# Two tiles of one expert's rows between attention and the expert loop, in place of one: picked from eight token tiles, their second matrix in plain float32

## The reference, cut to what matters

```python
scores = scale * q @ k.T, masked to 0 <= i - j < 64          # batch 4, heads 8, seq 576, head_dim 64
x = softmax(scores) @ v                                      # as x[2304, 512]
logits = x @ w_gate + log1p(exp(x @ w_noise)) * noise        # [2304, 8]
top2, top2_w = the two largest of each row, softmax over the two
for e in range(8):
    for k in range(2):
        mask = top2[:, k] == e
        h = np.maximum(x[mask] @ w1[e], 0.0)                 # w1[e]: 512 x 1024
        out[mask] += top2_w[mask, k, None] * (h @ w2[e])     # w2[e]: 1024 x 512
g = ramp(out @ w_in)                                         # 512 x 2048, piecewise quadratic
result = g @ w_out                                           # 2048 x 512
```

## Time and profile before

| | |
|---|---|
| time, median of 3 runs | 1076.76 us (1076.67 to 1077.49) |
| the profiled execution's own time | 1075.81 us |
| its span in the profile | 1073.8 us |
| mean granted TensorE clock | 0.998 |
| PE busy | 1054.0 us, 98% of the span |
| DVE, ACT, POOL busy | 344.5, 357.4, 392.9 us |

### The profile page before, as it was taken

How to read it: one execution, slowest core, us unless ns; L and a number is a source line. 1 busy time by engine, 2 the same in 40 slices (tenths; PEclk the granted TensorE clock), 3 DMA queues, 4 the chain that set the end, 5 groups by cost and what they waited for, 6 DMA issues and landing times.

```text
span 1073.8 us, 17646 instructions
## 1 busy us (share of the span) xinstructions
PE 1054.0 (98%) x5848; PEld 880.8 (82%) x5849; DVE 344.5 (32%) x695; ACT 357.4 (33%) x829; POOL 392.9 (37%) x309
## 2 busy tenths in 40 slices
PE   8999979999999999999999999999999999999998
PEld 6988758888888888888888887988888888888886
DVE  5878841122211221112221122332333332333222
ACT  4668532222222222222222221533344334335333
POOL 6233188785917255280552807830010000100000
PEclk9999999999999999999999999999999999999999
DMA  7685655949633324132241412240021002101001
GB/s 198 185 261 177 208 160 178 349 157 356 211 117 117 117 98 156 39 123 112 90 164 39 162 54 69 93 123 20 20 56 43 20 3 77 40 1 40 1 1 40
DMA packets 49282, 120.08 MB, mean 112 GB/s; under 512 B 6160, under 2 KB 11408, under 8 KB 48720
## 3 DMA queue, kind: packets, MB, share of 16 engines
q0 software_dynamic: 16688, 62.66, 17.7%
q1 hardware_dynamic: 19008, 32.62, 9.8%
q10 hardware_dynamic: 13536, 24.12, 6.6%
HBM read 86.88 MB, written 32.51 MB: 111 GB/s over the span
## 4 chain that ended last, share of the span: by engine, by line
PE 92%; DVE 2%; ACT 2%; DMA 1%; issue 1%; another core or an unknown queue 1%; ACTq 0%; POOL 0%; SPq 0%; DVEq 0%; POOLq 0%
PE bank L1521 7%; PE bank L1519 7%; PE bank L1520 7%; PE bank L1502 7%; PE bank L1504 7%; PE bank L1503 7%; PE bank L1567 6%; PE bank L1569 6%; PE bank L1568 6%; PE bank L1560 6%; PE bank L1562 6%; PE bank L1561 6%; PE bank L1527 3%; PE bank L1290 2%; PE bank L1486 2%; PE bank L1316 2%
## 5 line engine op out<-in xcount | busy, mean ns | idle before, releaser
L487 POOL TENSOR_TENSOR Wl<-stage,Wh 128x2048 fp32r<-128x2048 f32 x36 | 165.8, 4606 | 3.0
L1167 DVE COPY y_out<-bank 128x512 f32<-128x512 f32 x42 | 29.1, 692 | 353.8 <-PE bank L1521 353.8
L1502 PE MATMUL bank<-Wh,xT_h 128*128 x336 | 135.3, 403 | 1.3 <-issue 0.8
L1205 DVE SCALAR_TENSOR_TENSOR bank<-bank,square 128x512 f32<-128x512 f32 x72 | 50.4, 700 | 254.9 <-ACT square L839 254.9
L1504 PE MATMUL bank<-Wh,xT_l 128*128 x336 | 131.4, 391 | 0.0
L1521 PE MATMUL bank<-Wh,hT_l 128*128 x336 | 131.1, 390 | 0.0
L1519 PE MATMUL bank<-Wh,hT_h 128*128 x336 | 130.8, 389 | 0.1
L1520 PE MATMUL bank<-Wl,hT_h 128*128 x336 | 130.7, 389 | 0.0
L1503 PE MATMUL bank<-Wl,xT_h 128*128 x336 | 130.7, 389 | 0.0
L810 ACT ACTIVATE hT_h<-bank 128x512 fp32r<-128x512 f32 x84 | 45.7, 596 | 246.7 <-PE bank L1527 230.2
L485 POOL CAST Wh<-stage 128x2048 fp32r<-128x2048 f32 x36 | 68.5, 1904 | 157.9 <-PE bank L1521 156.5
(11 more groups left out here) (237 smaller groups left out, 1733.7 us busy)
## 6 DMA issues: line engine op xcount, KB each, us to landing
stage<-w POOLq DMA_DIRECT2D x32, 1024.0 KB
y_sorted<-y_out ACTq DMA_DIRECT2D x42, 256.0 KB
x_in<-x_sorted ACTq DMA_DIRECT2D x38, 256.0 KB
x_sorted<-gath_b SPq DMA_DIRECT2D x20, 256.0 KB
v_ring<-vW SPq DMA_DIRECT2D x36, 128.0 KB, 4.5
x_rows<-x_blk SPq DMA_DIRECT2D x36, 128.0 KB, 3.0
x_sorted<-gath_a SPq DMA_DIRECT2D x18, 256.0 KB
k_ring<-kT SPq DMA_DIRECT2D x8, 512.0 KB, 5.4
```

The costliest lines, as they stand in the source:

```text
L487: nc.gpsimd.tensor_tensor(Wl[:, s, cols], stage[:, c % 2], Wh[:, s, cols], ALU.subtract).then_inc(w_ready, 1)
L1502: nc.tensor.matmul(H_ps[a][:], xT_h[:, u, k], high, start=(k == 0), stop=False)
```

## The change

`EARLY` becomes 8 token tiles and the early tiles become two (`FIRST` = 2), of up to 256 rows of the star. `TILES` falls from 42 to 41, `ALL_TILES` stays 43.

- The steps of the early routing move from attention steps 13 to 26 to steps 20 to 35, with tiles twice as wide, four more matmuls in `early_ranks` and in `early_tokens` and a few more small operations. `BY_SCALAR` falls from 11 steps to 8, all of them even.
- The weights of the star are loaded from POOL's step 29 on (before: 23), w2 into a landing buffer of its own, `late_raw`. Only the 8 pieces of w1 are cast and split before routing; those of w2 are split after `find_tokens`, for the tiles of the loop.
- `early_out` multiplies with w2 as it landed: 8 matmuls in float32 for each of the two tiles, where it was 24 in fp32r for one. The hidden rows are copied once, without a low part.
- PE's order between attention and loop changes; all three fillers there are gone.
- The second expert's splitting waits for both early tiles to be stored and for all pieces of the star.

```diff
-BY_SCALAR = (15, 16, 17, 19, 20, 21, 22, 23, 26, 29, 32)
+BY_SCALAR = (20, 22, 24, 26, 28, 30, 32, 34)
+CASTS = {30: (0, 1), 31: (1, 2), 32: (2, 4), 33: (4, 5), 34: (5, 7), 35: (7, 8)}
+LOWS = {32: (0, 2), 34: (2, 4), 36: (4, 5), 37: (5, 6), 38: (6, 8)}
...
-    TILES = ALL_TILES - 1
+    FIRST = 2
+    TILES = ALL_TILES - FIRST
-    EARLY = E // 2
+    EARLY = E * FIRST // 2
...
+            late_raw = sb("late_raw", [P, 2 * STG])
+            e_hT = sb("e_hT", [P, FIRST, KF, P])
...
                 if t == GB:
-                    pool.wait_ge(ey_stored, 16)
+                    pool.wait_ge(ey_stored, 16 * FIRST)
+                    pool.wait_ge(w_ready, 4)
                     first_parts(1, 1, 1)
...
+            def early_hidden(b, first, after):
                 for i in range(first, after):
...
+                    if b == 0 and i in (0, KD):
+                        pe.wait_ge(w_ready, 1 + i // KD)
...
+            def early_out(b, first, after):
+                for k in range(first, after):
+                    if b == 0 and k % 4 == 0:
+                        pe.wait_ge(late_staged[k // 4], 16)
                     if k % 4 == 0:
-                        pe.wait_ge(ehl_ready, 1 + k // 4)
-                    cols = slice(KD * FF + D * k, KD * FF + D * k + D)
-                    for r, (h, w) in enumerate(((e_hT_h, Wh), (e_hT_h, Wl), (e_hT_l, Wh))):
-                        mm = nc.tensor.matmul(EY_ps[:], h[:, k], w[:, 0, cols], start=(k == 0 and r == 0),
-                                              stop=(k == KF - 1 and r == 2))
-                mm.then_inc(ey_done, 1)
+                        pe.wait_ge(ehT_copied, 2 * b + 1 + k // 4)
+                    mm = nc.tensor.matmul(EY_ps[b][:], e_hT[:, b, k], late_raw[:, D * k:D * k + D], start=(k == 0),
+                                          stop=(k == KF - 1))
...
                 if s == G + 1:
-                    pe.wait_ge(w_ready, 2)
-                    pe.wait_ge(exh_ready, 1)
-                    early_hidden(0, 2)
+                    early_transposes(1)
                 if s == G + 3:
-                    early_hidden(2, 4)
+                    early_hidden(0, 0, 4)
                 if s == G + 4:
-                    early_hidden(4, 8)
+                    early_hidden(0, 4, 8)
...
-            keep_busy(banks[0], 5)
+            early_hidden(0, 8, 24)
+            early_turn(0, 0)
+            early_hidden(1, 0, 12)
+            early_turn(0, 1)
             pe.wait_ge(route, ROUTE_PICKED)
...
-            early_out()
+            early_hidden(1, 12, 24)
+            pe.wait_ge(x_ready, G)
+            early_out(0, 0, 6)
...
-            keep_busy(banks[0], 8)
-            pe.wait_ge(tables_ready, 1)
-            pe.wait_ge(ey_copied, 1)
+            for a in range(2):
+                early_turn(1, a)
+            early_out(0, 7, 8)
...
+            early_out(1, 0, 4)
             transpose_x(0, 0, 0)
-            keep_busy(banks[0], 6)
+            early_out(1, 4, 8)
+            pe.wait_ge(tables_ready, 1)
+            pe.wait_ge(ey_copied, 1)
             tile_step(0, 0, 0)
```

More of the change, by code:

```diff
@@ L752, in _ @@
                 step(s)
-            for k in range(G + 4 - 24, 4 * PIECES):
-                cast_piece(k)
             act.wait_ge(route, ROUTE_NEGABS)
@@ L779, in _ @@
                 nc.scalar.activation(oh_lo[:, c], col_sq[:, k % 2], ACT.Relu, scale=-1.0, bias=1.0).then_inc(act_onehots, 1)
-            act.wait_ge(ey_done, 1)
-            nc.scalar.activation(e_y[:], EY_ps[:], ACT.Copy).then_inc(ey_copied, 1)
-            act.wait_ge(ey_copied, 1)
-            act.dma_start(y_sorted[0:P], e_y[:]).then_inc(ey_stored, 16)
+            for a in range(2):
+                early_turned(1, a)
+            for k in range(2 * PIECES, 3 * PIECES):
+                cast_piece(k)
+            early_y(0)
             act.wait_ge(ids_done, 1)
@@ L815, in tile_step @@
                     fetch(t + 4, u)
-            for u in range(2):
-                high_x(u, u)
+            high_x(0, 0)
+            for k in range(3 * PIECES, 4 * PIECES):
+                cast_piece(k)
+            early_y(1)
+            high_x(1, 1)
             act.wait_ge(y_cleared, 16 * (ALL_TILES - SURE))
@@ L1046, in step @@
                 early_step(s)
-                if 25 <= s < G:
-                    low_piece(s - 25)
+                for k in range(*LOWS.get(s, (0, 0))):
+                    low_piece(k)
             for s in range(G + 3):
@@ L1066, in _ @@
             nc.vector.memset(picked[:, NT], 0.0).then_inc(zeroed, 1)
-            for k in range(G - 25, 4 * PIECES):
-                low_piece(k)
+            early_then(nc.vector.tensor_tensor(order_eq[:], order_f[0:1].unsqueeze(2).to_broadcast([1, E, E]),
+                                               place[0:1, 0].unsqueeze(1).to_broadcast([1, E, E]), ALU.is_equal))
             dve.wait_ge(const_ready, ALL_CONSTANTS)
@@ L1146, in _ @@
             then(nc.vector.tensor_reduce(end_by_place[:], end_at[:], AX_X, ALU.add))
-            then(nc.vector.tensor_copy(last_tile[:], end_by_place[:]))
+            then(nc.vector.tensor_scalar(last_tile[:], end_by_place[:], 1.0 - FIRST, None, ALU.add))
             dve.wait_ge(route_act, 3)
```

240 lines of the change are left out of this document (131 added, 109 removed).

## The result

| | kernel before | changed kernel |
|---|---|---|
| time, median | 1077.12 us (1074.83 to 1078.03, 6 runs) | 1087.34 us (1083.98 to 1088.74, 6 runs) |
| the profiled execution | span 1073.8 | 1088.41, span 1086.8 |

The ratio is 1.0082 (95% interval 1.0065 to 1.01): 8.8 us slower by this ratio and 10.2 by the medians, where 8.7 us faster was forecast. The steps that the sum names for attention and for the stretch behind it can be found in the trace, most of them near their price. What is not in the sum is in the loop and the dense layer, whose instructions the change leaves as they were.

What follows compares the result with a forecast made beforehand. PE, busy 98%, was taken to bound the kernel, with DVE's routing chain and the gather bounding the stretch before the loop. -12.25 - 1.1 + 1.8 + 2.85 = -8.7 gave 1068.1 us, range 1065.2 to 1070.8.

Steps and rivals of the forecast that it cites:

- D: Rival: second expert's weights, started late by POOL, hold up the loop; 1083 at a slip to 190; chance 0.02.
- Part 1: Loop: one tile fewer, all tiles costing the same on PE; -12.25 us.
- Part 2: Attention: even steps no longer stalled, -1.5; more PE matmuls, +0.2; DVE's level steps, +0.2; in all -1.1 us.
- Part 3: Last scores to last logits: DVE's added pieces delay hidden matmuls, with the logits queued behind; +1.8 us, bounds 0.9 and 2.3.
- Part 4: Last logits to loop: float32 matmuls at 0.87 us fill PE's idle time; +2.85 us, bounds 0.4 and 3.5.
- rival A: Float32 matmuls ahead of the loop take two passes, 0.456 us each; that stretch +0.4, time 1065.6; chance 0.10.
- Part 5: Gathers in attention and the second expert's splitting cost nothing; gathers issued near 99.5 and 103.7, with 2.5 us margin.
- Rival E: PE's clock sinks under float32 work; 5 us at half rate would cost 2.5, 1070.6; chance 0.05.
- the forecast's case: The main sum holds: 1066.6 to 1069.8 us; chance 0.60.

Runs made afterwards that it cites:

- a1: The changed kernel with an unused 32-byte tensor behind `e_token`, restoring the loop's and dense layer's old SBUF addresses: 1064.39 us, again 1065.41 us.
- c4: a1 with the last logits put ahead of the four hidden matmuls `early_hidden(0, 4, 8)`: 1065.27 us, again 1064.87 us.
- b1: The kernel before without its unused 32-byte tensor `spare`, nothing else changed: 1097.11 us, ratio 1.0182.
- a3: The changed kernel with a 32-byte gap right ahead of `xT_h`, so only the loop's operands are back at multiples of 128 bytes: 1073.36 us.
- d1: a1 without `early_out(1, 0, 4)`, the first four of the second early tile's eight float32 matmuls: 1067.47 us.
- c1: The changed kernel with gaps ahead of `Wh` and the early tiles' tensors: `Wh`, `Wl` 32 bytes off, `xT`, `hT`, `gT`, `zT` at old places: 1084.39 us.
- e0: The changed kernel itself, run once more beside a1 on one chip: 1085.34 us.

## Why the prediction was wrong

**The step that failed** is the first one: "All tiles cost the same on PE", taken over from before to after, and with it the silent zero for the dense layer. Neither holds, since the change moved one operand of each of these matmuls by 32 bytes against the other. A tile takes 12.51 us in place of 12.25, which is 10.7 us over 41 tiles, and the dense layer 9 us more. None of the rivals was this. D, the only one that came out slower, had the second expert's weights; they did not hold anything up. In the changed kernel's trace POOL starts them at 156.51 (forecast 152), and PE's gaps in the loop are 0.25, 0.69 and 0.61 us, none of them put down to POOL or these weights.

**What was right** shows in a1, which is the change without the shifted addresses. The forecast was 1068.1 (1065.2 to 1070.8); a1 took 1064.39, which is 0.8 below the range, and 1065.41, which is in it. So even without the shift the kernel was 2.7 to 3.7 us faster than forecast. Its sum in spans (1063.0 against 1073.8):

| part | forecast | a1's trace against before's |
|---|---|---|
| the start, to the scores of step 4 | 0 | -1.17 (14.51 against 15.68) |
| 2, attention from there to step 35 | -1.1 | -1.39 (90.90 against 92.29) |
| 3, to the end of the last logits | +1.8 | +2.05 (14.30 against 12.25) |
| 4, to the loop's first matmul | +2.85 | +1.93 (27.68 against 25.75) |
| 1, one tile less | -12.25 | -12.25 |
| sum | -8.7 | -10.8 |

- *Part 1* holds if the addresses do.
- *Beside the spans*: against the runs of the kernel before on its own chip a1 gained 12.9 us. Of those the ones with a mean clock of 0.998 took 1075.28 to 1075.70, the ones with 0.994 took 1077.93 to 1080.17, and all four of a1 had 1.000. So some 2 us of the 12.9 go with the clock of the kernel before, which the forecast did not count.
- *Part 2*: the six even steps take 3.34 each, as said, and lost 1.7 us where 1.5 was counted; step 28 lost another 0.11. The two steps with PE's additional matmuls cost 0.24 and 0.20, twice the 0.2 of the sum. The 0.2 for DVE's level steps did not come: no other step is longer than 3.34. That the total is only 0.3 off is in part luck, since these misses offset each other.
- *Part 3*: the named waits are there, for `x_blk` (0.64) and for w1's second chunk (0.43), with the logits queued behind the latter. c4 moved them ahead and got the 1.8 us back for the logits, though only 0.7 to 0.9 for the loop.
- *Part 4* was 0.9 too dear. The float32 price was right (0.86 us measured, 0.87 forecast, where rival A had 0.46), and so was the way in which the old idle time was filled. The ranks start 7.24 us behind the logits' end (forecast 7.3), the search ends 19.2 behind it (forecast 19.3). Most of the rest is at the end. The last eight float32 records start from 144.35 on, 0.43 apart, so the eighth at 147.39, where the loop's first matmul (0.79 us long) starts too: that overlap is 0.4 us of the sum. And nothing is waited for with the tables.
- *Part 5*: the gathers were nearer to the edge than written. In the changed kernel POOL issued them at 97.79 and 105.39, with 6.54 us of waiting for the first one to land. PE turned the rows at 108.67 and 112.32 without a wait.
- *The start* was not in the sum. It differs from execution to execution: the scores of step 4 begin between 13.3 and 17.0 in the profiles here, in b1, which is the kernel before but for an address, at 17.01. In the two traces where they begin last (b1, and a3 at 16.29) the granted clock is 0.50 from 11.8 to 15.2, in that of the kernel before (15.68) it is not. The 1.17 us here are thus luck and no effect of the change that these runs could show.
- *Rival E* named float32 work as what could lower the clock. In the changed kernel's first profile it did sink, but among fp32r matmuls at 117, behind short waits, ahead of all float32 ones. In a1 it stays at 1.00 from 107 to 150, through all float32 matmuls there, and in d1 even behind a wait of 2.41 us. In the kernel before, with its idle 2.93 and 1.85 us, not one of the runs has a mean clock over 0.998.
- *The range of the forecast's case* (1066.6 to 1069.8) does not follow from the bounds of parts 2 to 4 taken singly; those give 1065.7 (part 4 at 0.4) to 1070.2 (part 2 at +1).

## What to carry to other kernels

A change of source that touches no instruction of a stage can still change its time, through where its operands lie. Compare the addresses of PE's operands in SBUF (the memory that they are read from) before and after any edit to the list of tensors, and give what is removed a placeholder when two versions are to be compared. For fp32r matmuls of 512 columns, the two operands had better lie alike: all fast ones here had both at the same place behind a multiple of 128 bytes. When a forecast takes a stage over as "the same", the first row to check afterwards is the distance between two matmuls in it. And where PE's work and a DMA are level, as here ahead of the loop, taking 3.5 us from PE alone gained 0.9.

## What the runs showed of the hardware

- An fp32r matmul of 512 columns starts 0.2267 to 0.2284 us behind the one before when both operands lie alike within 128 bytes (both at a multiple; or, in c1's early tiles, both 32 behind one), and 0.2333 (2.5% more) when the moving or the stationary one lies 32 or 96 bytes off against the other. At 64 bytes it is 0.2332 for the moving operand and 0.2301 for the stationary one (dense layer). The matmuls here are back to back; whether a PE that waits for others would show it was not tried.
- With 256 columns it is not a price: 0.1200 us with both alike, 0.1183 and 0.1167 with the moving one 96 and 32 bytes off. The float32 transposes of 128 columns, whose `hid` was shifted against `ident` in the changed kernel, take 1.03 to 1.04 us for eight, as before. Float32 matmuls of 512 columns with operands that lie differently were not tried.
- A float32 matmul of 512 columns leaves two records 0.43 us apart, 0.86 us in all: 3.8 times an fp32r one.
- The Trainium skill (FP8 and Floating Point Precision, TensorE Precision Notes) has four passes for it. At the fp32r distance for each pass that is an estimate of 0.91 us, and the trace's 0.86 is 6% below it.
- The granted clock fell to 0.50 for 6.8 us behind idle times of 0.61 and 0.43 us in one execution of the changed kernel; another (e0) passed the same place, with idle times of 0.64 and 0.43 us, at 1.00. In d1 it stayed at 1.00 behind 2.41 us.
